# Attention heads of a pair as separate matmuls in half of the array, with two score banks a block and one copy for both outputs

## What is computed

```python
scores = scale * np.matmul(q, k.transpose(0, 1, 3, 2))
mask_local = (rel >= 0) & (rel < stride)
mask_strided = (rel >= 0) & (pos[None, :] % stride == pos[:, None] % stride)
scores = np.where(masks[None, :, :, :], scores, -1000000000.0)
scores = scores - np.max(scores, axis=-1, keepdims=True)
attn = np.exp(scores)
attn = attn / (np.sum(attn, axis=-1, keepdims=True) + 1e-09)
return np.matmul(attn, v).astype(np.float32)
...
h = gelu(x @ w_in); u, v = halves of h
v_n = (v - mu) / np.sqrt(var + 1e-06) * g_ln
x = x + (u * (w_sg @ v_n + b_sg)) @ w_out
return x + relu(norm(x) @ w_ch1) @ w_ch2
```

## Time and profile before

| | us |
|---|---|
| median of 3 runs | 769.61 |
| lowest and highest | 767.61, 769.93 |
| span of the profiled execution | 766.5 |
| TensorE busy in it | 743.7 |
| VectorE busy | 345.1 |
| ScalarE busy | 283.1 |
| GpSimd busy | 201.2 |

### The profile page before, as it was taken

The page is one execution under the profiler, slowest core; times in us unless marked ns, Lnnn a source line. Parts: engine busy times, 40 slices in busy tenths (PEclk is TensorE's granted clock), DMA queues, the critical chain, the costliest instruction groups (busy, mean ns, idle before and its releaser), DMA issues.

```text
span 766.5 us, 14240 instructions
## 1 busy us (share of the span) xinstructions
PE 743.7 (97%) x5176; PEld 697.4 (91%) x5176; DVE 345.1 (45%) x787; ACT 283.1 (37%) x874; POOL 201.2 (26%) x208
## 2 busy tenths in 40 slices
PE   6798999999999999999999999999999999999998
PEld 4578986899689977999999999999999999999998
DVE  5955667635854485684453222321332223223212
ACT  6663458425943387343531212212112122121111
POOL 1518602530134203655450122111201220211000
PEclk9899999999999999999999999999999999999999
DMA  9525000600042001021420000000000000000000
GB/s 248 236 64 141 1 0 1 202 0 0 0 137 65 0 1 56 1 83 57 165 83 32 1 32 2 1 32 1 1 31 0 28 3 0 32 1 1 32 2 32
DMA packets 15373, 34.56 MB, mean 45 GB/s; under 512 B 1888, under 2 KB 6112, under 8 KB 15072
## 3 DMA queue, kind: packets, MB, share of 16 engines
q1 hardware_dynamic: 15328, 33.96, 14.0%
HBM read 29.23 MB, written 4.72 MB: 44 GB/s over the span
## 4 chain that ended last, share of the span: by engine, by line
PE 87%; issue 3%; DVE 3%; DMA 2%; ACT 2%; SPq 1%; POOL 1%; DVEq 0%; ACTq 0%; POOLq 0%
PE bank L821 26%; PE bank L823 26%; PE bank L822 26%; PE bank L867 3%; PE bank L842 2%; PE bank L853 2%; DMA win_raw<-w_in_dram 1%; DMA w_raw<-w_ff_dram 1%; ACT probs L461 1%; DVE stat L635 1%; PE bank L841 1%; SPq L257 1%; PE bank L926 1%; PE bank L925 1%; DVE res L652 0%
## 5 line engine op out<-in xcount | busy, mean ns | idle before, releaser
L784 DVE SCALAR_TENSOR_TENSOR hid_lo<-bank,hid_hi 128x288 fp32r<-128x288 f32 x128 | 58.5, 457 | 270.7 <-ACT hid_hi L591 270.6
L591 ACT ACTIVATE hid_hi<-bank 128x288 fp32r<-128x288 f32 x128 | 52.4, 410 | 288.5 <-PE bank L823 288.4
L821 PE MATMUL bank<-hid_hi,w_hi 128*128 128x288 f32 x512 | 151.1, 295 | 1.0 <-DVE hid_lo L784 1.0
L821 PE MATMUL bank<-xn_hi,w_hi 128*128 128x288 f32 x512 | 151.5, 296 | 0.6 <-DVE res L693 0.6
L823 PE MATMUL bank<-xn_hi,w_lo 128*128 128x288 f32 x512 | 151.7, 296 | 0.0
L822 PE MATMUL bank<-hid_lo,w_hi 128*128 128x288 f32 x512 | 151.1, 295 | 0.0
L823 PE MATMUL bank<-hid_hi,w_lo 128*128 128x288 f32 x512 | 150.9, 295 | 0.0
L822 PE MATMUL bank<-xn_lo,w_hi 128*128 128x288 f32 x512 | 150.2, 293 | 0.0
L821 PEld LDWEIGHTS bank<-hid_hi,w_hi 128*128 128x128 f32 x512 | 96.1, 188 | 1.2 <-issue 1.2
L821 PEld LDWEIGHTS bank<-xn_hi,w_hi 128*128 128x128 f32 x512 | 96.5, 189 | 0.8 <-DVE res L693 0.8
L822 PEld LDWEIGHTS bank<-xn_lo,w_hi 128*128 128x128 f32 x512 | 96.9, 189 | 0.0
(11 more groups left out here) (101 smaller groups left out, 1466.9 us busy)
## 6 DMA issues: line engine op xcount, KB each, us to landing
w_raw<-w_ff_dram SPq DMA_DIRECT2D x16, 512.0 KB, 3.5
k_sb<-kT_dram SPq DMA_DIRECT2D x32, 152.0 KB, 5.1
q_sb<-qT_dram SPq DMA_DIRECT2D x16, 288.0 KB, 5.8
out_dram<-res SPq DMA_DIRECT2D x7, 576.0 KB, 3.3
v_sb<-vW_dram SPq DMA_DIRECT2D x8, 384.0 KB, 5.0
v_sb<-vW_dram SPq DMA_DIRECT2D x8, 320.0 KB, 6.7
win_raw<-w_in_dram SPq DMA_DIRECT2D x4, 512.0 KB, 10.7
res<-w_sgT_dram SPq DMA_DIRECT2D x1, 1440.0 KB, 14.8
```

Of the source, the lines that this page charges most:

```text
L591: act.activation(hid_hi[:, f % 2, :], h_bank[f % 2][:, 0:HALF], ACT.Relu).then_inc(hh_ready, 1)
L784: dve.scalar_tensor_tensor(out=hid_lo[:, f % 2, :], in0=h_bank[f % 2][:, 0:HALF], scalar=0.0, in1=hid_hi[:, f % 2, :].bitcast(F32), op0=AL ...
L821: pe.matmul(dst, wh, xh, start=(start and i == 0), stop=False)
```

## The change

Each product of a pair becomes two, one for each head. For scores, head h takes rows 64 h to 64 h + 63 of q and k, so k_sb needs no zeros, no second copy and no memsets; each head writes its own bank, so a block takes two banks (2 (t % 2) and the next) instead of one of four. The mask is kept for one head and added by a matmul for each. For values, the weights of head h are its 64 columns of v and its output lies in partitions 64 h to 64 h + 63 of the same nq columns. Both outputs then lie below each other, and one copy on VectorE (copy_x, 128 partitions) takes the place of copy_low and copy_high.

With two slots for scores instead of four, the orders change too. TensorE makes scores(t+2) ahead of transposes(t), which wait for exps(t); two blocks instead of three are made ahead, between out groups 5 and 6. ScalarE has exps(t), copy_pT(t-3). VectorE has normalise(t-1), maxima(t), copy_x(t-5). The four pieces of the v product, one in each of the last four blocks before, stand now two by two in the last two.

```diff
-        k_sb = sb("k_sb", [P, PAIRS, 2, KPAD], F32, phase_a)
+        k_sb = sb("k_sb", [P, PAIRS, KPAD], F32, phase_a)
...
-            pool.memset(k_sb[0:D, 1:, 1, :], 0.0).then_inc(k_zero, 1)
...
-                for t in range(3, NT + 6):
-                    if 4 <= t < NT + 4:
-                        copy_pT(b, t - 4)
-                    if t >= 6:
-                        copy_high(b, t - 6)
+                for t in range(2, NT + 3):
                     if t < NT:
                         exps(b, t)
+                    if t >= 3:
+                        copy_pT(b, t - 3)
...
-                for t in range(3, NT + 6):
-                    if t >= 6:
-                        copy_low(b, t - 6)
+                for t in range(2, NT + 5):
+                    if t <= NT:
+                        normalise(b, t - 1)
                     if t < NT:
                         maxima(b, t)
-                    if t <= NT:
-                        normalise(b, t - 1)
+                    if t >= 5:
+                        copy_x(b, t - 5)
...
-                dst = s_bank[t % 4][0:nq, 0:2 * nk]
-                if t >= 4:
-                    pe.wait_ge(exp_done, b * NT + (t - 3))
+                dst = scores_at(t)
+                if t >= 2:
+                    pe.wait_ge(exp_done, b * NT + (t - 1))
...
-                pe.matmul(dst, eye_b[0:nq, 0:nq], mask, start=True, stop=False)
-                pe.matmul(dst, q_sb[:, pair, q0:q0 + nq], k_sb[:, pair, :, k0:k0 + nk],
-                          start=False, stop=True).then_inc(scores_ready, 1)
+                for h in range(2):
+                    pe.matmul(dst[:, h, :], eye_b[0:nq, 0:nq], mask_b[0:nq, m, 0:nk], start=True, stop=False)
+                for h in range(2):
+                    rows = slice(h * D, (h + 1) * D)
+                    last = pe.matmul(dst[:, h, :], q_sb[rows, pair, q0:q0 + nq], k_sb[rows, pair, k0:k0 + nk],
+                                     start=False, stop=True)
+                last.then_inc(scores_ready, 1)
...
-                pe.matmul(o_bank[t % 2][:, 0:2 * nq], v_sb[0:nk, t, :], probsT[0:nk, t % 2, 0:2 * nq],
-                          start=True, stop=True).then_inc(pv_ready, 1)
+                for h in range(2):
+                    rows = slice(h * D, (h + 1) * D)
+                    last = pe.matmul(o_bank[t % 2][rows, 0:nq], v_sb[0:nk, t, rows],
+                                     probsT[0:nk, t % 2, h * nq:(h + 1) * nq], start=True, stop=True)
+                last.then_inc(pv_ready, 1)
...
-                    if t + 3 < NT:
-                        scores(b, t + 3)
+                    if t + 2 < NT:
+                        scores(b, t + 2)
...
-                    if t >= NT - 4:
-
-                        v_part(b, t - (NT - 4), (0, 1))
+                    if t >= NT - 2:
+                        for s in range(2):
+                            v_part(b, 2 * (t - (NT - 2)) + s, (0, 1))
```

More of the change, by code:

```diff
@@ L64 @@
           + [("out", c, h) for h in range(2) for c in range(KC)])
-GROUP_BANK = [(NT - 4 + i) % 4 for i in range(4)] + [4] + 3 * list(range(8))
+GROUP_BANK = [0, 1, 2, 3, 4] + 3 * list(range(8))
 NGELU = NS + 2 * GC
@@ L150, in sequence_block_kernel @@
             w_lo.append(sb(f"w_lo{f}", [P, KC * P + DM], F32R))
-        bank = [ctx.enter_context(nc.psum_tensor(f"bank{i}", [P, 512], F32)) for i in range(8)]
-        s_bank, t_bank, o_bank = bank[0:4], bank[4:6], bank[6:8]
+        banks = ctx.enter_context(nc.psum_tensor("bank", [P, 8, 512], F32))
+        bank = [banks[:, i, :] for i in range(8)]
+        t_bank, o_bank = bank[4:6], bank[6:8]
         h_bank, mean_bank, var_bank, y_bank = bank[0:2], bank[2], bank[3], bank[4:8]
@@ L216, in res_chunks, with scores_at, heads_out @@
             return whole.rearrange("p (c t) -> p c t", c=KC)[:, :, first:first + n]
-        def head_out(b, t, low):
+        def scores_at(t):
+            _, nq, nk, _, _, _ = BLOCKS[t]
+            first = 2 * (t % 2)
+            return banks[0:nq, first:first + 2, 0:nk]
+        def heads_out(b, t):
             pair, nq, _, q0, _, m = BLOCKS[t]
-            p0, p1 = (0, D) if low else (D, P)
-            src = o_bank[t % 2][p0:p1, 0:nq] if low else o_bank[t % 2][p0:p1, nq:2 * nq]
+            src = o_bank[t % 2][:, 0:nq]
             if m != 2:
-                return res_at(b, pair, q0, nq, p0, p1), src
+                return res_at(b, pair, q0, nq), src
             r0, nr = q0 // CLASS, nq // CLASS
-            dst = res_at(b, pair, 0, S, p0, p1).rearrange("p (a r) -> p r a", r=STRIDE)[:, r0:r0 + nr, :]
+            dst = res_at(b, pair, 0, S).rearrange("p (a r) -> p r a", r=STRIDE)[:, r0:r0 + nr, :]
             return dst, src.rearrange("p (r a) -> p r a", a=CLASS)
@@ L254, in load_qkv @@
                         sp.dma_start(eye_f[:], eye).then_inc(mask_in, 16)
-                    for h in range(2):
-                        rows = slice(D * h, D * h + D)
-                        sp.dma_start(k_sb[rows, pair, h, :], kT[b, rows, pair, :]).then_inc(k_in[pair], 16)
+                    sp.dma_start(k_sb[:, pair, :], kT[b, :, pair, :]).then_inc(k_in[pair], 16)
                     blocks = slice(blocks_upto(pair - 1), blocks_upto(pair))
@@ L576, in batch @@
                         scale_q(b + 1, pair)
-                    for t in range(3):
+                    for t in range(2):
                         exps(b + 1, t)
             scale_q(0, 0)
-            for t in range(3):
+            for t in range(2):
                 exps(0, t)
@@ L767, in batch @@
                     add_out(b, i)
-                    if not last and 4 <= i <= 6:
-                        maxima(b + 1, i - 4)
-                        if i >= 5:
-                            normalise(b + 1, i - 5)
-            for t in range(3):
+                    if not last and 5 <= i <= 6:
+                        maxima(b + 1, i - 5)
+                        if i == 6:
+                            normalise(b + 1, 0)
+            for t in range(2):
                 maxima(0, t)
-                if t >= 1:
-                    normalise(0, t - 1)
+            normalise(0, 0)
             batch(0, first=True)
@@ L975, in batch @@
                     group(b, NGELU + NMIX + i)
-                    if not last and 4 <= i <= 6:
-                        scores(b + 1, i - 4)
+                    if not last and 5 <= i <= 6:
+                        scores(b + 1, i - 5)
             pe.wait_ge(const_ready, 2)
-            for t in range(3):
+            for t in range(2):
                 scores(0, t)
@@ L1059 @@
     lowest = np.float32(-1e9)
-    masks = np.full((P, 3, 2 * P), lowest, np.float32)
+    masks = np.full((P, 3, P), lowest, np.float32)
     row, col = np.arange(QB)[:, None], np.arange(P)[None, :]
```

52 lines of the change are left out of this document (18 added, 34 removed).

## The result

| | before | after |
|---|---|---|
| median us (lowest, highest) | 769.1 (767.61, 769.93) | 852.31 (851.35, 853.73) |
| span of the profiled execution | 766.5 | 850.6 |
| TensorE busy | 743.7 | 815.5 |
| mean granted clock | 0.99 to 1.00 | 0.918 |

The ratio is 1.1085, 95% interval 1.1067 to 1.1102. The prediction was 822 with a range of 810 to 850: the direction and the first mechanism were right, the size was not.

What follows compares the result with a forecast made beforehand. TensorE and ScalarE were nearly full in attention; VectorE's new order would set a 1.82 us chain per block. Batches 1 to 3 add 41.0 us, batch 0 11.6: 52.6 on 766.5 gives 819.1, median 822, range 810 to 850.

Steps and rivals of the forecast that it cites:

- The step that failed: Attention blocks: TensorE was taken to keep the upper clock at a steady 1.82 us a block, though no row showed it.
- TensorE has 0.6 us to spare in two blocks: Attention blocks: TensorE's path takes 3.05 us where two turns of VectorE's chain allow 3.64, so matmul changes lie beside it.
- The chain of 1.82 us a block: Every attention block: exponentials, reciprocal, multiply, maxima, next exponentials follow one another, 0.83 + 0.20 + 0.34 + 0.45 us, formerly spanning two blocks.
- GpSimd's stalls: Multiplies on the chain slowed by GpSimd subtractions: 8.2 us plus 0.95 in batch 0, 1.9 in each later batch.
- rival 3: GpSimd's stalls miss the multiply: the chain holds but 14.9 us of stalls fall elsewhere, 807 us; chance 0.06.
- The earlier start of batch 0: Batch 0: without k_sb memsets and with half the mask cast, first scores start 0.5 us earlier, exps(1) near 9.35.
- The v pieces behind transposes(20): End of each batch: four v pieces instead of two stand there, adding 2.74 us before values(20).
- rival 1: Attention blocks: TensorE's path becomes the longer chain at the 1.2 GHz clock, 846 us, with mode-change waits 865; chance 0.27.
- Rival 1's price: At the lower clock: 1.99 us a block, 13 us over 76 turns, plus 11 us for v product matmuls.
- The rival's side branch: Under rival 1, if the heads overlap, some 0.8 of the 3.98 us goes and the total is 825 to 833.
- Rival 4: Attention matmuls: the halves do not overlap, with the clock held high; same time as the forecast; no separate chance given.

## Why the prediction was wrong, step by step

- **The step that failed**: the forecast took the upper clock for a steady 1.82 us a block, and on it rests that TensorE has 0.6 us to spare in two blocks. Measured were 0.55, 0.54 and 0.55 in batches 1 to 3, 2.08 us a block, and 25.4 us more than the forecast's terms. The gap of 5.95 us, of which the prediction has no term, came on top and took the time out of the range: the same kernel with the two memsets that remove it takes 844.32.
- **The chain of 1.82 us a block**: right in each link. Its sum with this order alone is +41.7 us measured and 41.6 by the prediction's terms, but the batches differ: at values(20) they lose 10.9, 8.7, 10.9 and 11.3 us, where the terms give 8.8 and three times 10.9. The two GpSimd stalls that the terms have in each of batches 1 to 3 meet the chain there at none, one and two places. An agreement to 0.1 is luck.
- **GpSimd's stalls**: right in batch 0. There the four stalled multiplies of after last 2.4 to 2.5 us (2.40 and 2.42 at 32.88 and 38.51), as said; rival 3 is out. In each of batches 1 to 3 the first of the two subtractions met the multiply (1.57 to 1.67 us instead of 0.42) and the second missed it in batches 1 and 2, so about one stall of 0.95 a batch was charged too much.
- **The earlier start of batch 0**: wrong in after. exps(1) stand at 10.42, 0.6 later than before instead of 0.5 earlier; the first mask matmul waits for the keys' transfer until 7.77, before until 7.01. With the two memsets exps(1) stand at 9.43, near the 9.35 of the forecast, so this varies from one profile to another.
- **The v pieces behind transposes(20)**: right where the clock is high. From exps(21) to values(20) the prediction has 149.6 - 141.75 = 7.85 us; the kernel with both products over the whole array has 7.92, 7.84 and 7.89, and 9.51 where the clock was lower. In after it is 10.3 to 10.8.
- **"TensorE has 0.6 us to spare in two blocks"**: here the failed step enters the sum. It holds at 2.4 GHz and was computed along one path only. At 1.2 GHz the engine's own work in a block, 2.08 us, is more than the chain allows.
- **The chance of rival 1**: the prediction wrote of the clock that no row shows which level a steady 1.82 us a block would get, took the upper one as likeliest and gave the lower 0.27. For the new order alone this was nearly right, since with whole products 1.82 a block does keep the clock at 0.89 to 0.96; that the half-array products change this it did not consider. It weighed their speed alone.
- **Rival 1's price**: nearly right, 13 us for the pace and 11 for the tails. Measured beyond the forecast's own terms: to exps(21) 4.1 in each of batches 1 to 3 and 2.4 in batch 0, 14.8; in the tails 2.7 each and 2.4, 10.6. Together 25.4 against 24. With the gap of batch 2 (5.95) this is all but 0.2 of the 31.5 in 850.6 - 819.1. For the pace that is partly luck: the rival priced a path through three engines, 1.99 us a block, with TensorE waiting in it, and what set the pace was TensorE's own work, 2.08. The rival's side branch, that overlapping heads would bring it down to 825 to 833, failed: the heads do overlap at 1.2 GHz (values 0.52, scores 0.67), but the second mask matmul and the sum of all four steps keep TensorE above 1.82.
- **The gap**: unforeseen. Nothing in the trace of before shows one, and 6 us moved the time out of the range.
- **Rival 4**, that the halves bring nothing at full clock: true for the time. A block of scores takes 0.60 us in after (115.84 to 116.44) and 0.55 before, with its second mask; values take 0.31 instead of 0.35, and the transposes ahead of them 0.26 instead of 0.17.

Rows of after, PE, at full clock:

```profile
115.84 0.28 PE L826 MATMUL bank<-mask_b,eye_b 96*96 96x128 bf16 x2
116.05 0.46 PE L829 MATMUL bank<-k_sb,q_sb 64*96 64x128 f32 x4
116.44 0.40 PE L809 MATMUL bank<-op_hi,wout_hi 128*128 128x288 f32 x1
```

The Trainium skill, TensorEngine Tiling (Array Packing), section Overview, gives up to 2x for such dimensions. For matmuls this short the runs show 0.04 us for values at full clock, a tenth, and nothing for scores with their second mask; at 1.2 GHz values take 0.52 for 0.69 and scores without masks 0.67 for 0.91, about a quarter less. The same page of the Trainium skill, section Tiling Modes, says that a change of mode drains the engine; the 0.22 us of "issue" ahead of the weight loads of values, seen above at 1.2 GHz, and the transposes and masks that last longer ahead of a half product would fit, but no run here takes the changes of mode away by themselves.

## What to carry to other kernels

Before two steps on an engine's queue change places, walk the dependence through one turn of the loop: a step that waits for this block's result, put ahead of one that the next block needs, closes a chain that nothing hides. Where products are packed into parts of the array, or TensorE is left waiting, add up its work of one turn at 1.2 GHz too: that sum is the pace once the clock has fallen, and with both products halved it stayed down here for over 40 us a batch, where with whole ones it was back after about 7. Count also what the steps ahead of a half product lose, 0.09 to 0.19 us each here, before its gain is believed. An unexplained "issue" gap of some microseconds at a loop's start is worth a test with two idle instructions ahead of it before any theory is built on the time.

## What the runs showed of the hardware that was not expected

- The granted clock follows more than TensorE's busy time. It was 0.50 at 10.00 us busy of 10 with half-array products, and 0.96 at 35.97 of 43 with whole ones. Halved scores (half of the rows) weigh more than halved values (half of the columns): 0.71 to 0.74 against 0.80 to 0.89 when the other is whole. Whether rows weigh more than columns, or the longer product more than the shorter, is not separated, and what exactly the chip measures the runs do not say. Three bf16 matmuls of 384 columns put into each block held the clock for 22 and 24 us of two batches instead of 5, and then no more.
- Transposes and masks last longer ahead of a product in half of the array: transposes 0.26 instead of 0.17 us at full clock and 0.51 instead of 0.32 at 1.2 GHz, two masks 0.38 instead of 0.21 there. This takes back nearly all that the halves save.
- VectorE stood still for 5.95 to 6.13 us at one pass of its loop, in four of the twelve changed kernels, by where its code lay; two instructions ahead of it took the gap away.
